# Slot one-hots in 16 bits, eight tiles an instruction, in an attention and two-MoE kernel

## The reference

```python
# attention: a softmax over 7 taps weighs the token and the 6 before it
w = softmax(weight_gen)                       # batch, seq, 8 heads, 7 taps
x[b, s, h] = sum_k w[b, s, h, k] * x_pad[b, s + k, h]
# first MoE: 8 experts, two of them for each token
noisy = x @ w_gate + log1p(exp(x @ w_noise)) * noise
top2, their softmax weights g0, g1
out[n] = sum over the two: g * (relu(x[n] @ w1[e]) @ w2[e])    # 192 -> 1024 -> 192
# second MoE: cosine scores against 8 expert embeddings, the best expert alone
e = argmax(normalized(x) @ normalized(expert_emb).T / tau)
out[n] = softmax(scores)[e] * (relu(x[n] @ w1[e]) @ w2[e])
```

## Time and profile before

| What | Value |
| --- | --- |
| time, median of 3 runs | 1212.66 us (1211.81 to 1212.79) |
| the profiled execution | 1213.03 us |
| its span | 1211.2 us |
| TensorE, VectorE, ScalarE, GpSimd busy | 92%, 61%, 47%, 43% of the span |
| TensorE's share of the chain that ended last | 82% |

### The profile page before, as it was taken

One profiled execution on the slowest core, in us unless ns is written; L12 is line 12 of the kernel. 1 busy time (PEld: TensorE's weight loads), 2 busy tenths in 40 slices (PEclk: granted clock), 3 DMA queues, 4 the chain that ended last, 5 costly groups with the idle time before them and its releaser, 6 DMA issues.

```text
span 1211.2 us, 28336 instructions
## 1 busy us (share of the span) xinstructions
PE 1109.2 (92%) x8013; PEld 1058.0 (87%) x8013; DVE 735.7 (61%) x1462; ACT 565.1 (47%) x1615; POOL 518.9 (43%) x726
## 2 busy tenths in 40 slices
PE   1889288999999999999999999979489999999997
PEld 0556176999999999999999999979479999999997
DVE  8999695556565655656556565431855665567663
ACT  2121285445454544545445454346544554456553
POOL 5888002444444444444444444400034444444444
PEclk9999689999999999999999999955589999999999
DMA  9444471313131131312213131189421313124511
GB/s 324 123 105 120 97 3 30 90 39 98 41 91 51 42 103 39 95 39 78 65 42 94 42 103 39 39 290 226 34 72 55 101 43 98 39 70 122 143 57 37
DMA packets 90935, 103.61 MB, mean 86 GB/s; under 512 B 31475, under 2 KB 76379, under 8 KB 90620
## 3 DMA queue, kind: packets, MB, share of 16 engines
q1 hardware_dynamic: 72828, 67.36, 24.0%
q0 software_dynamic: 18048, 35.52, 10.6%
HBM read 69.72 MB, written 34.69 MB: 86 GB/s over the span
## 4 chain that ended last, share of the span: by engine, by line
PE 82%; DVE 8%; POOL 3%; DMA 2%; issue 2%; ACT 2%; POOLq 0%; SPq 0%; DVEq 0%
PE banks L672 22%; PE banks L674 10%; PE banks L658 9%; PE banks L660 7%; PE banks L664 7%; PE banks L659 7%; PE banks L663 7%; PE banks L588 4%; PE banks L598 3%; DVE prods L940 2%; POOL prods L468 2%; PE banks L642 2%; PE banks L643 2%; PE banks L578 2%; PE banks L634 2%
## 5 line engine op out<-in xcount | busy, mean ns | idle before, releaser
L1114 DVE SCALAR_TENSOR_TENSOR h_lo<-banks,h_hi 128x256 fp32r<-128x256 f32 x736 | 312.3, 424 | 334.4 <-ACT h_hi L835 330.8
L835 ACT ACTIVATE h_hi<-banks 128x256 fp32r<-128x256 f32 x736 | 282.9, 384 | 419.0 <-PE banks L664 418.9
L672 PE MATMUL banks<-w_hl,h_hi 128*128 128x384 f32 x1472 | 465.8, 353 | 0.0
L674 PE MATMUL banks<-w_hl,h_lo 128*128 128x192 f32 x1472 | 367.5, 250 | 0.0
L674 PEld LDWEIGHTS banks<-w_hl,h_lo 128*128 128x128 f32 x1472 | 279.4, 190 | 0.0
L672 PEld LDWEIGHTS banks<-w_hl,h_hi 128*128 128x128 f32 x1472 | 276.6, 188 | 0.2
L480 POOL DMA_INDIRECT x_slots<-token_rows,gather_idx x192 | 190.4, 992 | 112.3 <-POOL gather_idx L473 81.9
L658 PE MATMUL banks<-x_hi_a,w_hi 128*128 (+1 forms) x736 | 226.4, 308 | 1.1 <-DVE x_hl_b L1074 0.8
L664 PE MATMUL banks<-x_hl_b,w_lo 128*128 (+1 forms) x736 | 207.2, 282 | 0.0
L659 PE MATMUL banks<-x_hi_a,w_lo 128*128 (+1 forms) x736 | 207.0, 281 | 0.0
L660 PE MATMUL banks<-x_lo_a,w_hi 128*128 (+1 forms) x736 | 206.6, 281 | 0.0
(11 more groups left out here) (165 smaller groups left out, 1362.4 us busy)
## 6 DMA issues: line engine op xcount, KB each, us to landing
raw<-in_moe_w SPq DMA_DIRECT2D x17, 768.0 KB
token_rows<-stage SPq DMA_DIRECT2D x28, 384.0 KB, 5.6
choices<-choice_rows SPq DMA_DIRECT2D x28, 384.0 KB, 5.0
raw<-in_moe_w SPq DMA_DIRECT2D x17, 512.0 KB
raw<-in_moe_w SPq DMA_DIRECT2D x34, 256.0 KB
x_halo<-in_x SPq DMA_DIRECT2D x2, 2688.0 KB, 15.4
token_rows<-rows SPq DMA_DIRECT2D x14, 384.0 KB, 13.2
x_slots<-token_rows,gather_idx POOLq DMA_INDIRECT x192
```

What stands on the lines that cost most here:

```text
L672: mm(y[:, i, 0:2 * D], h_hi[:, c % HBUFS, t], w2_hl[u][:, c, :, :], start=c == 0, stop=False)
L674: ins = mm(y[:, i, 0:D], h_lo[:, c % HBUFS, t], w2_hl[u][:, c, 0, :], start=False, stop=c == FC - 1)
L835: sc.activation(h_hi[:, c % HBUFS, :], banks[:, c % HBANKS, 0:BLOCK], ACT.Relu).then_inc(h_hi_ready[m], 1)
L1114: v.scalar_tensor_tensor(h_lo[:, c % HBUFS, :], banks[:, c % HBANKS, 0:BLOCK], 0.0, h_hi[:, c % HBUFS, :].bitcast(F32), ALU.max, ALU.subtr ...
```

## The change

`ONEHOTS` is 8 in place of 4. The one-hots and the scaled high ones are bf16 tiles with the tile number innermost: `[P, columns, 8]`. Low and high one-hot are two instructions in both layers and have a semaphore each. ScalarE scales the first four tiles of a group, VectorE the other four in one product with `row_code`. TensorE takes its operands with a step of eight elements and waits for both.

A row number is no longer an integer in float form. A code is `CODE_MIN + 128 * t + p`, and the 16 bits of the code are read as a bf16 number: sign and exponent and fraction. Each slot gets one such number, added to zeros, so that the upper half of the 32-bit sum is the code again. VectorE shifts it down, takes off `CODE_MIN`, and has the gather row. For this the rows of `token_rows` are numbered tile by tile (`tile_rows`): row t * 128 + p, where before they were in the order of tokens. `choice_rows` is numbered p * 112 + t (`choice_view`), and `store_rows` is worked out from partition and tile in further steps. The gates of a choice are stored by one DMA of 7,168 numbers, where there were two of 3,584. On GpSimd `column_no` is filled eight times as wide, and the codes are made in three instructions.

```diff
-ONEHOTS = 4
+ONEHOTS = 8
+HOTS_ACT = 4
+CODE_MIN = 71 * 128
...
-        column_no = sb("column_no", [P, P], BF16)
+        column_no = sb("column_no", [P, P, ONEHOTS], BF16)
-        row_no = sb("row_no", [P, CHOICES[0] * T])
-        signed_row = sb("signed_row", [P, B, J])
+        row_code_i = sb("row_code_i", [P, CHOICES[0] * T], I32)
+        row_code = sb("row_code", [P, CHOICES[0] * T], BF16)
...
+        tile_rows = lambda a, t, n: a.rearrange("(t p) d -> p t d", p=P)[:, t:t + n]
+        choice_view = lambda t, n: choice_rows.rearrange("(p t) d -> p t d", p=P)[:, t:t + n]
...
# SP
-                    sp.dma_start(token_view(token_rows[0][k * N:(k + 1) * N])[b, :, jj * GROUP:(jj + 1) * GROUP, 0:D],
-                                 stage[g % 2][:]).then_inc(rows_stored[g % 2], 16)
+                    sp.dma_start(tile_rows(token_rows[0], k * T + g * GROUP, GROUP)[:, :, 0:D], stage[g % 2][:]).then_inc(rows_stored[g % 2], 16)
...
-                    for b in range(B):
-                        sp.dma_start(token_view(token_rows[m][k * N:(k + 1) * N])[b, :, :, D:D + 1],
-                                     gate[k][:, b * J:(b + 1) * J].unsqueeze(2), allow_slow_non_contiguous=True).then_inc(gates_stored[m], 16)
+                    sp.dma_start(tile_rows(token_rows[m], k * T, T)[:, :, D:D + 1], gate[k][:].unsqueeze(2),
+                                 allow_slow_non_contiguous=True).then_inc(gates_stored[m], 16)
...
# GpSimd
+            gp.iota(row_code_i[:], [[P, CHOICES[0] * T]], base=CODE_MIN, channel_multiplier=1).then_inc(consts_step, 1)
+            pool.wait_ge(consts_step, 3)
+            gp.tensor_scalar(row_code_i[:], row_code_i[:], 65536.0, None, ALU.mult).then_inc(consts_step, 1)
+            pool.wait_ge(consts_step, 4)
+            gp.tensor_copy(row_code[:], row_code_i[:].bitcast(F32)).then_inc(consts_ready, 1)
...
# TensorE
+                    pe.wait_ge(hots_ready[m], g + 1)
+                    pe.wait_ge(dve_rows_ready[m], g + 1)
                     pe.wait_ge(hi_rows_ready[m], g + 1)
                     for i in range(ONEHOTS):
-                        ins = mm(banks[:, 2, 0:cols], hots[m][g % HOT_BUFS][:, 1, i, :], hi_rows[m][g % HOT_BUFS][:, i, 0:cols],
+                        ins = mm(banks[:, 2, 0:cols], hots[m][g % HOT_BUFS]["lo"][:, :, i], hi_rows[m][g % HOT_BUFS][:, :, i],
...
# ScalarE
-                    for i in range(ONEHOTS):
+                    for i in range(HOTS_ACT):
                         t = g * ONEHOTS + i
-                        ins = sc.activation(hi_rows[m][g % HOT_BUFS][:, i, 0:cols],
-                                            hots[m][g % HOT_BUFS][:, 0, i, 0:cols].bitcast(F32), ACT.Copy, scale=row_table[m][:, t:t + 1])
+                        ins = sc.activation(hi_rows[m][g % HOT_BUFS][:, :, i], hots[m][g % HOT_BUFS]["hi"][:, :, i], ACT.Copy,
+                                            scale=row_code_i[:, t:t + 1].bitcast(F32))
...
# VectorE
+                    v.tensor_tensor(hot["hi"][:], column_no[:, 0:cols, :],
+                                    slot_hl[:, 0, tiles].unsqueeze(1).to_broadcast([P, cols, ONEHOTS]), ALU.is_equal).then_inc(hi_hots_ready[m], 1)
+                    v.tensor_tensor(hot["lo"][:], column_no[:],
+                                    slot_hl[:, 1, tiles].unsqueeze(1).to_broadcast([P, P, ONEHOTS]), ALU.is_equal).then_inc(hots_ready[m], 1)
+                    dve.wait_ge(hi_hots_ready[m], g + 1)
+                    codes = row_code[:, g * ONEHOTS + HOTS_ACT:(g + 1) * ONEHOTS]
+                    v.tensor_tensor(hi_rows[m][u][:, :, HOTS_ACT:], hot["hi"][:, :, HOTS_ACT:],
+                                    codes.unsqueeze(1).to_broadcast([P, cols, ONEHOTS - HOTS_ACT]), ALU.mult).then_inc(dve_rows_ready[m], 1)
...
+                step(v.tensor_scalar(q["id_code"], banks[:, 2, 0:cols].bitcast(I32), 16, None, ALU.logical_shift_right))
+                v.tensor_scalar(gather_rows[:, 0:cols], q["id_code"], float(-CODE_MIN), 0.0, ALU.add, ALU.max).then_inc(ids_ready[m], 1)
+                dve.wait_ge(ids_ready[m], 1)
+                step(v.tensor_scalar(q["id_part"], gather_rows[:, 0:cols], P - 1, None, ALU.bitwise_and))
+                step(v.tensor_scalar(q["id_tile"], gather_rows[:, 0:cols], P.bit_length() - 1, None, ALU.logical_shift_right))
```

More of the change, by code:

```diff
@@ L70, in attention_moe_moe @@
     assert B == 2 and S % P == 0 and J % GROUP == 0 and D == P + 64 and F % P == 0 and E % 2 == 0
-    assert LAG == FC % HBANKS and K == 7 and max(HI_COLS) <= P and S <= 1 << 12 and max(MAXB) < 256 and GHALF <= 512 and CHOICES[0] * T < 256
-    assert PAD_ROW > CHOICES[0] * N
+    assert LAG == FC % HBANKS and K == 7 and max(HI_COLS) <= P and CHOICES[0] * T <= P and CHOICES[1] * T % ONEHOTS == 0 and max(MAXB) < 256 and GHALF <= 512 and CHOICES[0] * T < 256
+    assert PAD_ROW > CHOICES[0] * N and CODE_MIN + P * CHOICES[0] * T < 255 * P
     token_rows = [nc.dram_tensor(f"token_rows{m}", (CHOICES[m] * N, ROW), F32, kind="Internal").ap() for m in range(2)]
@@ L178, in attention_moe_moe @@
         hots, hi_rows = [], []
-        for m, kind in enumerate((F32, F32R)):
+        for m in range(2):
             with ExitStack() as routing:
-                hots.append([sb(f"hots{m}_{u}", [P, 2, ONEHOTS, P], kind, routing) for u in range(HOT_BUFS)])
-                hi_rows.append([sb(f"hi_rows{m}_{u}", [P, ONEHOTS, max(HI_COLS)], kind, routing) for u in range(HOT_BUFS)])
-        sb("hots_space", [P, HOT_BUFS, 2 * ONEHOTS * P + ONEHOTS * max(HI_COLS)])
+                hots.append([{"lo": sb(f"hots{m}_{u}_lo", [P, P, ONEHOTS], BF16, routing),
+                              "hi": sb(f"hots{m}_{u}_hi", [P, HI_COLS[m], ONEHOTS], BF16, routing)} for u in range(HOT_BUFS)])
+                hi_rows.append([sb(f"hi_rows{m}_{u}", [P, HI_COLS[m], ONEHOTS], BF16, routing) for u in range(HOT_BUFS)])
+        sb("hots_space", [P, HOT_BUFS, (P + 2 * max(HI_COLS)) * ONEHOTS // 2])
         idf = {n: sb(n, [P, max(HI_COLS)]) for n in ("id_second", "id_pad", "id_row")}
+        idi = {n: sb(n, [P, max(HI_COLS)], I32) for n in ("id_code", "id_tile", "id_part")}
         consts_step = sem("consts_step")
@@ L231, in attention_moe_moe @@
         table_ready = [sem(f"table_ready{m}") for m in range(2)]
+        hi_hots_ready = [sem(f"hi_hots_ready{m}") for m in range(2)]
+        dve_rows_ready = [sem(f"dve_rows_ready{m}") for m in range(2)]
         hots_ready = [sem(f"hots_ready{m}") for m in range(2)]
@@ L396, in _ @@
                 for k in range(2):
-                    src = token_view(choice_rows[k * N:(k + 1) * N])
                     sp.dma_start(choices[g % CHOICE_BUFS][:, k, :].rearrange("p (j d) -> p j d", d=D),
-                                 src[b, :, jj * GROUP:(jj + 1) * GROUP, :]).then_inc(choices_in[g % CHOICE_BUFS], 16)
+                                 choice_view(k * T + g * GROUP, GROUP)).then_inc(choices_in[g % CHOICE_BUFS], 16)
             for g in range(NG):
-                b, jj = divmod(g, GB)
                 sp.wait_ge(rows_ready[1], g + 1)
-                sp.dma_start(token_view(token_rows[1])[b, :, jj * GROUP:(jj + 1) * GROUP, 0:D],
-                             rows[:, g * GROUP:(g + 1) * GROUP, :]).then_inc(x1_stored, 16)
+                sp.dma_start(tile_rows(token_rows[1], g * GROUP, GROUP)[:, :, 0:D], rows[:, g * GROUP:(g + 1) * GROUP, :]).then_inc(x1_stored, 16)
             sp.wait_ge(gates_ready[1], 1)
@@ L429, in _ @@
                              pattern=[[1, P]], channel_multiplier=-1)
-            gp.iota(column_no[:], [[1, P]], base=0, channel_multiplier=0, allow_small_or_imprecise_dtypes=True)
+            gp.iota(column_no[:], [[1, P], [0, ONEHOTS]], base=0, channel_multiplier=0, allow_small_or_imprecise_dtypes=True)
             gp.iota(expert_rank[:], [[-1, E]], base=E, channel_multiplier=0, allow_small_or_imprecise_dtypes=True)
[L432 to L436, removed]
+            gp.iota(row_code_i[:], [[P, CHOICES[0] * T]], base=CODE_MIN, channel_multiplier=1).then_inc(consts_step, 1)
[3 more added lines that the diff above has]
+            gp.tensor_copy(row_code[:], row_code_i[:].bitcast(F32)).then_inc(consts_ready, 1)
             def first_lo(c):
@@ L554, in _ @@
             mixture(0, choice_rows, CHOICES[0] * N - 1,
-                    [(rows_stored[u], 32 * (NG // 2)) for u in range(2)] + [(gates_stored[0], 16 * B * CHOICES[0])])
-            mixture(1, out, N - 1, [(x1_stored, 16 * NG), (gates_stored[1], 16 * B)])
+                    [(rows_stored[u], 32 * (NG // 2)) for u in range(2)] + [(gates_stored[0], 16 * CHOICES[0])])
+            mixture(1, out, N - 1, [(x1_stored, 16 * NG), (gates_stored[1], 16 * CHOICES[1])])
         @block.tensor
@@ L845, in hot_rows @@
             def hot_rows(m):
[L847 removed]
                 for g in range(CHOICES[m] * T // ONEHOTS):
[L849 removed]
+                    act.wait_ge(hi_hots_ready[m], g + 1)
                     if g >= HOT_BUFS:
```

(20 more changed lines are left out.)

4 lines of the change are left out of this document (removed).

## The result

The changed kernel takes 1204.95 us in the median of 6 runs (1203.78 to 1206.88), the kernel before 1212.49 (1210.63 to 1213.14): a ratio of 0.9941, with a 95% interval of 0.9928 to 0.9954. It is faster by 7.5 us, where 20 were forecast, and it lies outside the forecast's range.

What follows compares the result with a forecast made beforehand. VectorE was taken to pace layer one's slot one-hots, ScalarE layer two's. From 1213.03 us, 14.2 (layer one) and 5.9 (layer two) came off: 1192.9, set to 1192.6 since that execution stood 0.4 above the median; range 1189.5 to 1199.5.

Steps and rivals of the forecast that it cites:

- VectorE, two elements a cycle: Layer one's one-hots and products: 16-bit operands run at two a cycle, 1.63 us a group, 22.8 us for fourteen.
- ScalarE ... 0.29 us a piece behind the first, 1.28 a group, covered by VectorE's 1.63: Layer one: ScalarE scales four of eight tiles in 1.28 us a group, hidden behind VectorE, which sets the pace.
- the threshold, 0.35 us more a group: Layer one: ScalarE becomes the bound if its strided 16-bit reads cost over 0.35 us more a group.
- the case a chance of 0.07: Rival: ScalarE or TensorE above 1.63 us a group; 2 to 5 us lost, 1195 to 1198; chance 0.07.
- TensorE ... 0.105: One-hot groups: eight single bf16 passes replace 16, each taken as 0.105 us at 1.2 GHz.
- my upper end of 0.21: TensorE's pass with no gain: 0.21 us, 1.7 a group, so 1 us in 14 groups and 0.85 in the last.
- In layer two the wait on the gate store takes the place of the wait on the row numbers: Layer two's index copy: gates land 8.85 us behind readiness, copy at 876.4 not 882.32, 5.9 us gained, not 7.9.
- The rival of later gates: Both layers' gate stores land later, 3.6 and 3.7 us behind the row numbers; 1193 to 1200, middle 1197; chance 0.17.
- the forecast's 176.5: Layer one's index copy at 176.5 in place of 190.66, 14.2 us earlier, with the gates there 2.3 us before.
- Clock: First products' start: layers one and two swap 2.4 and 1.2 GHz, so 0.9 us swaps places, bounds 0.9 either way.
- Constants: GpSimd's start: wider column_no and three row-code instructions cost 1.5 to 3 us more, covered by 5.86 us idle.

Runs made afterwards that it cites:

- the rows of single instructions: The changed kernel with single ScalarE copies and TensorE passes, strided or dense, added behind its end; some 40 us longer by the added work, time not compared.

## Why the prediction was wrong

*VectorE, two elements a cycle:* right to the hundredth (0.69 and 0.42 us); where nothing held it a group took 1.54 us (148.67 to 150.21), 1.63 in the sum. The bytes per cycle read from today's two-input row led to the right rate. The Trainium skill, "VectorE: DVE Perf Modes", section "The perf-mode tier table", gives tensor_tensor twice the rate for bf16 in SBUF, and the trace agrees: 1,024 elements in 0.69 us.

*"ScalarE ... 0.29 us a piece behind the first, 1.28 a group, covered by VectorE's 1.63":* this is the step that failed. I priced an instruction whose output changed from dense fp32 to 2-byte elements 16 bytes apart by the row of the old form. It took 0.59 us a piece, 2.35 a group: 0.72 x 14 = 10 us of the 10.8 that layer 0 fell short. Taking two or all tiles off ScalarE gave back 7.0 and 6.9 us of the stretch, and there TensorE's own mis-sized term took over; writing densely, which relieves both engines, gave back 9.7. The text even named the threshold, 0.35 us more a group, though for the strided reads, and then gave the case a chance of 0.07 and 2 to 5 us. The excess was 1.07 us, and most of it was the strided writes'.

*"TensorE ... 0.105":* mis-sized too. It took 0.236, over my upper end of 0.21, since the moving operand's step costs it (0.24 us against 0.07 in the rows of single instructions). Behind ScalarE this showed only in the last group (2.06 us for 0.85); once ScalarE alone is relieved it is the bound at 1.89 a group.

*"In layer two the wait on the gate store takes the place of the wait on the row numbers":* right in mechanism, wrong in size. The copy comes 11.3 us behind the gates and not 8.85; this is 2.4 us, and layer 1's miss is 2.2. The rival of later gates came nearer for layer 1 (the copy 17.8 us behind the first one-hot; 16.3 measured, 14.1 forecast), but by luck: it took the store to change, and neither the addresses nor the number of DMAs moved it. The same misreading is in layer 0, where the gates were to land 2.3 us ahead of the row numbers, at 174.2. Before the change they landed at 176.6, so the forecast's 176.5 had no slack, and with dense output the store is indeed last there.

*Clock:* 0.70 gained and 1.23 lost where 0.9 and 0.9 were written; only one of the two starts had the low clock. *Constants:* GpSimd's took 1.93 us for the wide one and lay in the idle time, as forecast.

*The attention stage, 2.0 us earlier:* nothing ties it to the change. It was not in the forecast, and it varies between kernels whose attention code is the same. The windows of 60 to 90 us (us, busy of PE, PEld, DVE, ACT, POOL with counts, granted clock, DMA share, GB/s) of the kernel before, of the changed one and of the one with two tiles on ScalarE:

```profile
60.00:90.00 30.00, 26.21 (x120) 17.81 (x118) 28.50 (x17) 7.29 (x18) 25.47 (x17) 0.94 0.44 106
```

```profile
60.00:90.00 30.00, 26.13 (x123) 17.32 (x122) 29.40 (x18) 7.03 (x17) 26.64 (x18) 1.00 0.35 106
```

```profile
60.00:90.00 30.00, 26.12 (x120) 17.84 (x119) 28.50 (x16) 7.29 (x18) 25.49 (x17) 0.94 0.35 106
```

Where TensorE's clock dips there (0.94), the first one-hot comes at 149.9 to 150.6 us, where it doesn't at 148.6 to 148.8 (kernels that finish the gates behind the third group); both kinds occur among the kernels with the change. What makes it dip in one and not in the other stays open.

Of the profile's 8.7 us, then, 7.1 lie in the two routing stretches, and the two clock swaps give back 0.5.

## What to carry to other kernels

Price an instruction by its access pattern as well as by its count of elements: a layout that doubles one engine's rate is read and written by the others too, and here it nearly doubled ScalarE's time for a piece (0.33 to 0.62 us) and more than tripled TensorE's pass (0.067 to 0.24). When a wait is about to become the last one, take its time from where it lands and not from where its traffic fades. A rival whose threshold lies near the forecast (0.35 us of slack) deserves a larger chance and a place in the range, even if no row prices it.

## What the runs showed of the hardware

- ScalarE, 128 bf16 elements: 0.33 us a piece dense, 0.43 with input at a step of 16 bytes, 0.62 with output at that step. In fp32 the output's step costs 0.03 us.
- TensorE, 128 bf16 columns at 2.4 GHz: 0.067 us a pass dense, 0.24 with the moving operand at a step of 16 bytes; at 1.2 GHz the latter is 0.236, so the reading and not the clock sets it.
- Layer 1's 7,168 stores of 4 bytes land 10.5 to 12.7 us behind their issue, layer 0's 14,336 about 20 to 24. For the 7,168, two halves (11.6 behind the second issue) against one store (11.1), and steps of 772 bytes (12.4) against 98,816 (11.1), show no difference beyond that spread. The last packets of the kernel before show some 2.4 us ahead of the landing (876.3 and 878.6 us in layer 1, 174.2 and 176.6 in layer 0).
